# Attention, MoE and gated MLP in one kernel: a shorter centroid chain, another order of the first inverses, fewer zero matmuls at the start

## The reference

```python
q_n = q / (norm(q) + 1e-6); k_n = ...; c_n = centroids / (norm(centroids) + 1e-6)
q_assign = argmax(q_n . c_n); k_assign = argmax(k_n . c_n)       # 16 centroids per head
scores = 0.125 * q @ k.T where q_assign == k_assign, else -1e9
attn = exp(scores - max); attn = attn / (sum(attn) + 1e-9);  x = attn @ v
...
h = x @ w_in; P = a0 + a1 h + a2 h^2 + a3 h^3; Q = 1 + |b0| |h| + |b1| h^2
x = (P / (Q + 1e-6)) @ w_out
...
out = (silu(x @ w_gate) * (x @ w_val)) @ w_out2
```

## Time and profile before

| | |
|---|---|
| median of 3 runs | 779.73 us (779.42 to 779.96) |
| the profiled execution's own time | 780.16 us |
| its span, first to last instruction | 778.3 us |
| TensorE busy | 772.1 us, 99% of the span, 4219 matmuls |
| VectorE / ScalarE / POOL busy | 565.0 / 522.0 / 522.8 us |
| DMA | 57.53 MB, mean 74 GB/s |

### The profile page before, as it was taken

How to read it: one execution, slowest core, us unless ns; L and a number is a source line. 1 busy time by engine, 2 the same in 40 slices (tenths; PEclk the granted TensorE clock), 3 DMA queues, 4 the chain that set the end, 5 groups by cost and what they waited for, 6 DMA issues and landing times.

```text
span 778.3 us, 12686 instructions
## 1 busy us (share of the span) xinstructions
PE 772.1 (99%) x4219; PEld 699.2 (90%) x4219; DVE 565.0 (73%) x1010; ACT 522.0 (67%) x996; POOL 522.8 (67%) x457
## 2 busy tenths in 40 slices
PE   8999999999999999999999999999999999999998
PEld 8899999999998888888888888899999999999997
DVE  6999999999998787777777777644544555554554
ACT  6889888988888787686767789553554444333322
POOL 5679999997575997222222488879888975665610
PEclk9999999999999999999999999999999999999999
DMA  8757665463402600000000111342212204111002
GB/s 187 189 147 182 165 176 139 118 163 91 120 14 82 189 1 1 1 0 1 1 0 1 28 44 39 95 122 55 55 28 55 55 29 135 55 41 42 27 1 82
DMA packets 57521, 57.53 MB, mean 74 GB/s; under 512 B 6576, under 2 KB 44272, under 8 KB 57456
## 3 DMA queue, kind: packets, MB, share of 16 engines
q1 hardware_dynamic: 57296, 56.32, 27.0%
q10 hardware_dynamic: 160, 0.39, 0.2%
HBM read 33.59 MB, written 3.15 MB: 47 GB/s over the span
## 4 chain that ended last, share of the span: by engine, by line
PE 97%; ACT 1%; DVE 1%; DMA 0%; issue 0%; ACTq 0%
PE ps L1344 19%; PE ps L1346 19%; PE ps L1345 19%; PE ps L1499 8%; PE ps L1518 4%; PE ps L1520 4%; PE ps L1442 4%; PE ps L1443 4%; PE ps L1441 4%; PE ps L1487 4%; PE ps L1473 4%; PE ps L1552 2%; ACT prob L917 1%; PE ps L1451 0%; DMA cen<-in_centroids 0%
## 5 line engine op out<-in xcount | busy, mean ns | idle before, releaser
L609 POOL TENSOR_TENSOR den<-den,mag 128x512 f32<-128x512 f32 x48 | 62.3, 1298 | 118.5 <-ACT den L790 118.3
L668 POOL TENSOR_TENSOR w_lo<-w_raw,w_hi 128x768 fp32r<-128x768 f32 (+1 forms) x48 | 101.7, 2127 | 56.4 <-ACT w_hi L849 56.4
L1346 PE MATMUL ps<-x_hi,w_lo 128*128 128x512 f32 (+1 forms) x384 | 139.4, 363 | 0.0
L1344 PE MATMUL ps<-x_hi,w_hi 128*128 128x512 f32 (+1 forms) x384 | 139.1, 362 | 0.0
L1345 PE MATMUL ps<-x_lo,w_hi 128*128 128x512 f32 (+1 forms) x384 | 139.1, 362 | 0.0
L1251 DVE TENSOR_TENSOR probT_lo<-ps,probT_hi 128x384 fp32r<-128x384 f32 x192 | 97.8, 551 | 9.4 <-ACT probT_hi L937 8.2
L690 POOL TENSOR_SCALAR prob<-prob,row_inv 128x768 f32<-128x768 f32 x96 | 85.7, 907 | 27.7 <-DVE row_inv L1241 26.7
L937 ACT ACTIVATE probT_hi<-ps 128x384 fp32r<-128x384 f32 x192 | 83.5, 487 | 17.9 <-PE ps L1499 15.1
L1230 DVE TENSOR_REDUCE neg_max<-ps 128x1 f32<-128x768 f32 x96 | 90.7, 946 | 2.0 <-PE ps L1487 1.5
L917 ACT ACTIVATE prob<-ps,neg_max 128x768 f32<-128x768 f32 x96 | 86.6, 902 | 2.1 <-DVE neg_max L1230 2.0
L1499 PE MATMUL ps<-ident,prob 128*128 128x128 f32 x576 | 79.8, 274 | 0.3 <-DVE probT_lo L1251 0.3
(11 more groups left out here) (150 smaller groups left out, 1990.6 us busy)
## 6 DMA issues: line engine op xcount, KB each, us to landing
w_raw<-in_moe_w_gate SPq DMA_DIRECT2D x48, 128.0 KB, 2.3
w_raw<-in_moe_w_val SPq DMA_DIRECT2D x48, 128.0 KB, 2.6
k_hihi<-qk_hi SPq DMA_DIRECT2D x31, 192.0 KB, 3.3
w_raw<-in_moe_w_in SPq DMA_DIRECT2D x16, 256.0 KB, 3.7
w_raw<-in_moe_w_out SPq DMA_DIRECT2D x16, 256.0 KB, 4.5
qk_raw<-in_q SPq DMA_DIRECT2D x16, 192.0 KB, 4.0
qk_low<-qk_hi SPq DMA_DIRECT2D x16, 192.0 KB, 3.7
qk_low<-qk_lo SPq DMA_DIRECT2D x16, 192.0 KB, 4.1
```

The costliest lines, as they stand in the source:

```text
L668: did(g.tensor_tensor(lo[:, wave, :], raw[:, wave, :], hi[:, wave, :].bitcast(F32), ALU.subtract), s_w2lo)
L1344: mm(dst, hi, m_hi, start=start, stop=False)
L1346: return mm(dst, lo, m_hi, start=False, stop=stop)
```

## The change

It touches three places.

1. The centroid chain: a small constant, 1e-36, is added under the square root as the activation's bias, from a column of `cs` that VectorE sets; ScalarE waits for that (`s_guard`). The guard by a maximum is gone, two steps are one (`scalar_tensor_tensor`), so that four steps are left. The high parts `cen_hh` are written by VectorE, not ScalarE.
2. The first inverses: for tile 0 VectorE adds the two columns of `row_sum` itself by a reduction, and ScalarE's `denominators` skips it. For tiles 1 and 2 (step 3) the inverses move from behind the maximum to a place between head 2's `sum_logit` and `top_logit`.
3. `WARM_CEN` is 14, not 19.

```diff
-    EPS_NORM, EPS_SUM = 1e-6, 1e-9
+    EPS_NORM, EPS_SUM, SQUARE_MIN = 1e-6, 1e-9, 1e-36
...
-    WARM_CEN, WARM_CENT, WARM_LOGIT, WARM_TOP = 19, 6, 4, 5
+    WARM_CEN, WARM_CENT, WARM_LOGIT, WARM_TOP = 14, 6, 4, 5
...
             sc.wait_ge(s_cen_v, 2)
-            s.activation(cs[:, 1:2], cs[:, 0:1], ACT.Sqrt).then_inc(s_cen_a, 1)
+            sc.wait_ge(s_guard, 1)
+            s.activation(cs[:, 1:2], cs[:, 0:1], ACT.Sqrt, bias=cs[:, 6:7]).then_inc(s_cen_a, 1)
             s.preload_act_table_set("natural_log_exp_and_others")
-            sc.wait_ge(s_cen_v, 8)
-            s.activation(cen_hh[:, 0:3:2, :].bitcast(F32R), cen[:, :].unsqueeze(1).to_broadcast([P, 2, D]),
-                         ACT.Identity, scale=cs[:, 7:8]).then_inc(s_cen_hh, 1)
...
             def denominators(step):
                 half, cols = den_at(step)
-                if half is not None:
+                if half is not None and cols.stop > 1:
                     sc.wait_ge(s_eps, 1)
-                    sc.wait_ge(s_exp, HALF * (half + 1) if half else cols.stop)
+                    sc.wait_ge(s_exp, HALF * (half + 1))
...
+            v_.memset(cs[:, 6:7], SQUARE_MIN).then_inc(s_guard, 1)
             ve.wait_ge(s_cen_in, 16)
...
             ve.wait_ge(s_cen_a, 1)
-            then(v_.tensor_scalar(cs[:, 2:3], cs[:, 1:2], 1e-30, None, ALU.max))
-            then(v_.reciprocal(cs[:, 3:4], cs[:, 2:3]))
-            then(v_.tensor_tensor(cs[:, 4:5], cs[:, 0:1], cs[:, 3:4], ALU.mult))
-            then(v_.tensor_tensor(cs[:, 5:6], cs[:, 4:5], cs[:, 1:2], ALU.add))
-            then(v_.tensor_scalar(cs[:, 6:7], cs[:, 5:6], 0.5, EPS_NORM, ALU.mult, ALU.add))
-            then(v_.reciprocal(cs[:, 7:8], cs[:, 6:7]))
+            then(v_.reciprocal(cs[:, 2:3], cs[:, 1:2]))
+            then(v_.scalar_tensor_tensor(out=cs[:, 3:4], in0=cs[:, 2:3], scalar=cs[:, 0:1], in1=cs[:, 1:2],
+                                         op0=ALU.mult, op1=ALU.add))
+            then(v_.tensor_scalar(cs[:, 4:5], cs[:, 3:4], 0.5, EPS_NORM, ALU.mult, ALU.add))
+            then(v_.reciprocal(cs[:, 5:6], cs[:, 4:5]))
+            v_.tensor_scalar(cen_hh[:, 0:3:2, :].bitcast(F32R), cen[:, :].unsqueeze(1).to_broadcast([P, 2, D]),
+                             cs[:, 5:6], None, ALU.mult).then_inc(s_cen_hh, 1)
             ve.wait_ge(s_cen_hh, 1)
...
-                    n = inverse_count(half, cols)
                     if half >= 2:
                         ve.wait_ge(s_norm, HALF * (half - 1))
-                    ve.wait_ge(s_den, n)
+                    if cols.stop == 1:
+                        ve.wait_ge(s_eps, 1)
+                        ve.wait_ge(s_exp, 1)
+                        v_.tensor_reduce(row_den[:, cols], row_sum[:, cols, :], AX.X, ALU.add).then_inc(s_den_0, 1)
+                        ve.wait_ge(s_den_0, 1)
+                    else:
+                        ve.wait_ge(s_den, half + 1)
                     v_.reciprocal(row_inv[:, cols], row_den[:, cols]).then_inc(s_inv, 1)
...
-                late = step > T
+                late = step > T or step == FIRST_DEN + 1
                 if not late:
                     inverses(step)
...
-                if late:
+                if late and step > T:
                     inverses(step)
...
                 if h is not None:
                     sum_logit(h)
+                    if step == FIRST_DEN + 1:
+                        inverses(step)
                     top_logit(h)
```

More of the change, by code:

```diff
@@ L238, in build_program @@
         "s_zeros", "s_gap", "s_topz", "s_scale", "s_const", "s_row0", "s_par", "s_bneg", "s_eps", "s_early"))
+    s_guard = sem("s_guard")
     s_cen_a, s_cen_v, s_cen_hh, s_cen_ll, s_cen_t, s_cen = (sem(x) for x in (
@@ L244, in build_program @@
         "s_logit", "s_top", "s_istop", "s_topT", "s_topT_in", "s_rank", "s_cluster"))
-    s_score, s_max, s_exp, s_den, s_inv, s_norm = (sem(x) for x in (
-        "s_score", "s_max", "s_exp", "s_den", "s_inv", "s_norm"))
+    s_score, s_max, s_exp, s_den, s_den_0, s_inv, s_norm = (sem(x) for x in (
+        "s_score", "s_max", "s_exp", "s_den", "s_den_0", "s_inv", "s_norm"))
     s_pT, s_pT_hi, s_pT_lo, s_pv, s_xhi, s_xlo = (sem(x) for x in (
@@ L1080, in _ @@
                                     in0=cen[:, :].unsqueeze(1).to_broadcast([P, 2, D]),
-                                    scalar=cs[:, 7:8], in1=cen_hh[:, 0:3:2, :],
+                                    scalar=cs[:, 5:6], in1=cen_hh[:, 0:3:2, :],
                                     op0=ALU.mult, op1=ALU.subtract).then_inc(s_cen_ll, 1)
```

## The result

The changed kernel takes 780.74 us (median of 22 executions), the kernel before 779.67 (22 executions, 779.31 to 780.20). The medians are 1.07 us apart, a ratio of 1.0014, and the means 1.86 us. The ratio taken over all executions is 1.0025 with a 95% interval of 1.0017 to 1.0033: slower, by a quarter of one per cent. The forecast was 779.35, a gain of 0.38 us on the 779.73 measured then.

What follows compares the result with a forecast made beforehand. TensorE was taken to bound nearly the whole kernel except the start, up to 26.47 us. Centroid chain -0.40 and inverses +0.02 gave -0.38 us, applied as 779.73 to 779.35 us; range 778.8 to 780.6.

Steps and rivals of the forecast that it cites:

- the sum: Whole kernel: centroid chain -0.40 plus moved inverses 0.02 gives -0.38 us, with the clock's rise unmoved; chance 0.50.
- The rival of a late clock: TensorE from 6.7 us to the second logits: the clock rises later, kernel slower, 780.4 to 780.9; chance 0.25.
- The 14 zeros: TensorE's start: zeros end 1.15 us earlier, no gain by itself; idling grows from 0.42 to 1.2, rise taken unmoved.
- The rival's price: Late clock at zeros and logits: 0.70 us slower, or 1.18 if the second twelve logit matmuls also run low; chance 0.25.
- the added memset: Guard constant set on VectorE while it waits for the centroids: claimed to cost nothing, since that engine is idle.
- cenT 0.40 earlier: Centroid chain at the start: ScalarE's copy cenT moves from 7.01 to 6.61 us, and the logits from 7.76 to 7.36.
- What reaches TensorE's last gap: TensorE's last idle gap, ending at 26.47 us: the change is worth only the time its work there comes earlier.
- The inverses at nothing: ScalarE before logit_lo: dropping one row_den frees 0.18 us, but logit_lo gains 0.04 at most, so taken as nothing.
- the third rival: Inverses worth more: if ScalarE releases logit_lo, 0.18 us is handed on and root additions cost nothing, 779.0; chance 0.12.
- The reciprocal's 0.02: VectorE: the second inverse, moved behind head 2's sum of logits, costs 0 to 0.17 us, taken as 0.02.
- The transfers: Rival: head 0's copies or head 1's k hold the scores, gain 0 to 0.3 us, 779.4 to 779.7; chance 0.13.
- Faster 0.03, slower 0.04: Whole kernel: chances of a distinguishable gain or loss, no case reaching 1.56 us either way.

Runs made afterwards that it cites:

- run 1: The changed kernel with 19 warm-up zeros instead of 14, nothing else: 780.43 us, ratio 1.0011 to the kernel before.
- run 9: The changed kernel with its 14 zeros and one more idle VectorE memset: 779.85 us, ratio 1.0020 to the kernel before.
- run 2: The kernel before with 14 zeros instead of 19, nothing else: 783.75 us, ratio 1.0048.
- run 8: The changed kernel with 17 zeros and one more idle VectorE memset: 779.14 us, ratio 0.9991 to the kernel before.
- run 10: The changed kernel with 12 zeros, started late to pass into the transposes without a gap, and one more VectorE memset: 779.95 us, ratio 1.0004 to the kernel before.
- run 7: The changed kernel with 19 zeros and one more idle VectorE memset: 779.43 us, ratio 0.9993 to the kernel before.
- run 5: The kernel before with one more small VectorE memset in idle time: 780.71 us, ratio 1.0015.
- run 6: The kernel before with two more small VectorE memsets in idle time: 779.47 us, ratio 0.9996.
- run 12: Repetition of the changed kernel with 17 zeros and one more VectorE memset: 778.95 us, ratio 0.9992 to the kernel before.
- run 11: The changed kernel with 17 zeros, no bias under the root or wait for it, and two small VectorE memsets: 779.16 us, ratio 0.9995 to the kernel before.

## Why the prediction was wrong

The forecast had a small gain, its range reached 780.6, and the median is 780.74. Two steps failed: a cost of 1.2 us that the sum did not have at all, and the clock's rise, taken "where it is now". Either alone would have left the median inside the range (run 1: 780.43, run 9: 779.85), though as a loss. The rival of a late clock, chance 0.25, named the right mechanism of the second, and its 780.4 to 780.9 holds the median by luck: that price is neither group's. Step by step:

- **The 14 zeros**, "In the sum I take the rise where it is now": this step failed, in five of 22 executions (five of 12 in run 9, five of 6 in run 2). Run 2 shows it alone, runs 8 and 10 that closing the gap cures it.
- **The rival's price**, 0.70 to 1.18 us, was too small. A logit matmul at the low level takes 0.20 (2.40 / 12), not my 0.165. More than that, I let the clock come back by the second group, and it stayed low until 17.4 us, over both groups and the rank matmuls. From the centroids' landing to the first exponential it is 16.25 us instead of 12.29, or 3.96 later although cenT is 0.27 earlier. Against run 1, where it is 12.04, the low clock costs 4.2 us up to there, which is most of the 4.7 between the low and the late group.
- **What no step had**: the place of instruction fetches. The changed kernel has one VectorE instruction more. That costs 0.9 in the last store and 0.3 at the gate in each of the three profiles with that count, and 1.0 and 1.2 in the medians (run 1 against 7, run 5 against 6). I had put the added memset at nothing because VectorE is idle there; its own time is nothing, its place in the stream is not. This alone is larger than all the terms of my sum.
- **cenT 0.40 earlier**: 0.25 to 0.27 measured, in the profiles that compare best. The distance from landing to cenT scatters by as much: 3.46 to 3.82 in five profiles with the old chain, 3.17 to 3.45 in eight with the new one (without run 10). The root took 0.29 as forecast, and cen_hh on VectorE 0.29, not 0.35. The term failed in the distance: I timed cenT from cen_ll, 0.68 ahead. The four transposes are one block of 1.08 us from the release by cen_hh (5.64 to 6.72 in the chain), and cen_ll was never what they waited for. Timed from the end of cen_hh, 1.15 ahead of cenT before, the same numbers give 6.67, and 6.65 with its measured end of 5.50; the other 0.11 is that the block ran wholly at the low level (1.08 against 0.97).
- **What reaches TensorE's last gap**, the measure I had named: counted from VectorE's first operation on the centroids, it is 23.04 us in the kernel before and 22.60 to 22.86 in the six profiles of the whole change with an early rise (runs 1, 7, 8, 9, 12, and 11, which lacks only the bias), so 0.2 to 0.4 earlier. The gain of 0.38 was there, about as forecast, and the two steps above hid it.
- **The inverses at nothing**: 0.19 arrived between the exponentials, as the third rival had it. I read TensorE's matmul at 18.69 as head 2's last logit. The twelve matmuls of that step are six of head 2 and then six of head 3's first half (FOURTH has its logits start at step 3). The last of head 2's starts at 18.02 and is shown to 18.30, well ahead of logit_lo at 18.93, so ScalarE's own order, not TensorE, released logit_lo, and the 0.18 was handed on. The reciprocal's 0.02 measured as nothing.
- **The transfers** held nothing; their margins were enough.
- **"Faster 0.03, slower 0.04"** rested on no case reaching 1.56 us. A loss of some 1.2, which run 9 takes from the low and the late group alike, and one of 4.7 in five of 22 bring the means 1.86 apart; the medians, 1.07 apart, stay under it.

## What to carry to other kernels

A kernel that unrolls thousands of instructions should be compared with itself plus one idle instruction before a difference of a microsecond is put down to an edit: here one memset in idle time moved the time by 1.0 us, and a second one moved it back. Filler matmuls are there to leave TensorE no long idle stretch before the clock has risen, measured against the latest landing of the data and not the usual one; look at the spread over executions, not at one profile or a median. And when a matmul is said to release something, count which iteration of the code it belongs to.

## What the runs showed of the hardware

- **The fetch of instructions is not always hidden.** When one falls into the last store, one share of it, by my reading that of one of sixteen DMA engines, is 0.8 us late, and the store lands after 3.07 instead of 2.17 us. Near 556 us, 0.7 us ahead of another fetch, a VectorE operation whose semaphore has been seen starts 0.35 late in the same three profiles. The Trainium skill (Runtime: NRT & Kernel Launch, section "Instruction fetch mechanics") calls the cost of crossing into the next block mostly hidden. Here the measurement decides: 0.9 and 0.3 us of it are not.
- **The clock.** With 17 or 19 zeros the rise lies (from the 1.2 GHz level to 2.4 GHz, by the pace of the matmuls) between 4.0 and 6.8 us over ten profiles; after an idle stretch of 1.12 us it came at 17.4, after one of 0.65 us (run 2) at 16.6, after one of 0.22 us (run 9) at 5.8. The late ones came although TensorE worked nearly without a pause from 5.6 (5.2) on. The Trainium skill (TensorE: Matmul & The Clock Gate, section "Part 1: The HAM clock gate") says that the place varies from run to run, and these runs agree: the ten profiles have it 2.8 us apart, and of twelve executions of one kernel (run 9), five are some 4.9 us slower than six others.
- **The clock can fall again.** In run 6 the granted clock is 0.5 (1.2 GHz) for 3.4 us from 18.75 us on, with TensorE as busy ahead of it as in a kernel whose clock stayed. Executions with a mean granted clock of 0.998, eleven of 97 of the kernel before, take some 1.2 us more.
- **The landing of the first load varies** by 0.9 us (2.5 to 3.4 us from the first instruction) over fourteen profiles. Times at the start only compare when counted from it.
